# A turn in front of TensorE's attention loop that steps over its body, with six stretches of it under a condition on the counter

## The reference

```python
for t in range(S):
    cur = np.einsum('bhd,bhe->bhde', u[None] * kt, vt)
    y[:, :, t] = np.einsum('bhd,bhde->bhe', rt, state + cur)
    state = w[None, :, :, None] * state + np.einsum('bhd,bhe->bhde', kt, vt)
```

## Time and profile before

| what | value |
|---|---|
| median of 3 runs | 616.07 us (615.64 to 616.73) |
| profiled execution | 615.47 us |
| its span, first to last instruction | 613.7 us |
| mean granted TensorE clock | 0.996 |
| TensorE busy | 596.3 us, 97% |
| VectorE, ScalarE, GpSimd busy | 291.8, 227.6, 145.4 us |
| instruction packets | 29 on q8, 0.48 MB; 12 on q14, 0.10 MB |

### The profile page before, as it was taken

How to read it: one execution, slowest core, us unless ns; L and a number is a source line. 1 busy time by engine, 2 the same in 40 slices (tenths; PEclk the granted TensorE clock), 3 DMA queues, 4 the chain that set the end, 5 groups by cost and what they waited for, 6 DMA issues and landing times.

```text
span 613.7 us, 17314 instructions
## 1 busy us (share of the span) xinstructions
PE 596.3 (97%) x7377; PEld 533.0 (87%) x7377; DVE 291.8 (48%) x462; ACT 227.6 (37%) x409; POOL 145.4 (24%) x177
## 2 busy tenths in 40 slices
PE   6789999999999999999999999999999999999997
PEld 6689999766999999999688888888898888888886
DVE  5578898196677777774121332232132133223212
ACT  3256666434655555552321222132132122213212
POOL 6567887235055332221230000000000000000000
PEclk9899999999999999999999999999999999999999
DMA  7679997595566777640400030030011001001001
GB/s 134 129 150 185 185 184 194 199 321 210 175 240 260 280 273 266 225 148 20 162 1 0 1 104 0 1 103 1 1 51 52 1 1 52 0 1 51 1 0 52
DMA packets 103673, 67.77 MB, mean 110 GB/s; under 512 B 79124, under 2 KB 97688, under 8 KB 103632
## 3 DMA queue, kind: packets, MB, share of 16 engines
q1 hardware_dynamic: 76288, 57.89, 30.9%
q10 hardware_dynamic: 25552, 4.72, 4.1%
q0 software_dynamic: 1792, 4.58, 2.1%
HBM read 55.92 MB, written 12.19 MB: 111 GB/s over the span
## 4 chain that ended last, share of the span: by engine, by line
PE 50%; DVE 0%; ACT 0%; issue 0%
PE gl_pab L1518 32%; PE gl_po L1533 8%; PE p_pair L1533 8%; PE gl_pab L1506 1%; PE p_pair L93 0%; DVE gl_g_lo L1600 0%; DVE gl_g_sb L1598 0%; ACT gl_g_hi L1578 0%; ACT gl_a_sb L1575 0%; DVE gl_o_sb L1611 0%
## 5 line engine op out<-in xcount | busy, mean ns | idle before, releaser
L1598 DVE TENSOR_TENSOR gl_g_sb<-gl_a_sb,gl_pab 128x512 f32<-128x512 f32 x48 | 33.0, 688 | 186.3 <-ACT gl_a_sb L1575 186.3
L1518 PE MATMUL gl_pab<-gl_xT_hi,wm_lo 128*128 128x512 f32 x288 | 112.9, 392 | 0.0
L1518 PE MATMUL gl_pab<-gl_xT_lo,wm_hi 128*128 128x512 f32 x288 | 112.8, 392 | 0.0
L1518 PE MATMUL gl_pab<-gl_xT_hi,wm_hi 128*128 128x512 f32 x288 | 112.1, 389 | 0.0
L1575 ACT ACTIVATE gl_a_sb<-gl_pab 128x512 f32<-128x512 f32 x48 | 28.7, 597 | 183.9 <-PE gl_pab L1518 183.9
L1518 PEld LDWEIGHTS gl_pab<-gl_xT_hi,wm_lo 128*128 128x128 f32 x288 | 54.0, 188 | 11.4
L1518 PEld LDWEIGHTS gl_pab<-gl_xT_hi,wm_hi 128*128 128x128 f32 x288 | 54.1, 188 | 10.6 <-DVE gl_xT_lo L1605 0.3
L1518 PEld LDWEIGHTS gl_pab<-gl_xT_lo,wm_hi 128*128 128x128 f32 x288 | 54.0, 188 | 10.5
L1275 PE MATMUL ex_ph<-ex_xT_hi,ew_w_hi 128*128 128x224 f32 x192 | 52.9, 275 | 0.0
L1275 PE MATMUL ex_ph<-ex_xT_hi,ew_w_lo 128*128 128x224 f32 x192 | 52.7, 274 | 0.0
L1275 PE MATMUL ex_ph<-ex_xT_lo,ew_w_hi 128*128 128x224 f32 x192 | 52.7, 274 | 0.0
(11 more groups left out here) (204 smaller groups left out, 1220.9 us busy)
## 6 DMA issues: line engine op xcount, KB each, us to landing
w_in<-in_moe_w SPq DMA_DIRECT2D x8, 1536.0 KB, 8.1
ew_w_in<-in_moe_w SPq DMA_DIRECT2D x8, 1536.0 KB, 6.5
w_in<-in_moe_w SPq DMA_DIRECT2D x14, 512.0 KB, 7.3
k_in<-in_k SPq DMA_DIRECT2D x48, 96.0 KB
v_in<-in_v ACTq DMA_DIRECT2D x48, 96.0 KB
r_in<-in_r SPq DMA_DIRECT2D x48, 96.0 KB
w_in<-xbuf SPq DMA_DIRECT2D x12, 384.0 KB, 3.8
out<-gl_o_sb SPq DMA_DIRECT2D x12, 384.0 KB, 2.4
```

What stands on the lines that cost most here:

```text
L1518: m = pe.matmul(p_ab[f % 2][w][:, :], a[:, w * KD + k, cols], b[t.slot][:, k, :], start=(k == 0 and n == 0), stop=(k == KD - 1 and n == 2))
L1598: dve.tensor_tensor(g_sb[f % 2][:, :], a_sb[f % 2][:, :], p_ab[f % 2][1][:, :], ALU.mult).then_inc(s_g, 1)
```

## The change

TensorE's loop gets seven turns instead of six. In the turn with c = 0 its body is not run: six stretches of it stand under `pe.If(c > 0)`. Two things that stood ahead of the loop move into that turn, under `pe.If(c < 1)`: the key powers, behind the fourth stretch, and the first tile's transposes with their three waits, at the turn's end. In the other turns the counter is one more than before; so BASE and the initial counts of the semaphores for v grow with it, on all engines, and the waits' constants too. The other engines' loops stay as they are.

```diff
-        BASE = 4
+        BASE = 8
...
-                wait(pe, s_vin[t.slot], t.chunk(32, 64))
+                wait(pe, s_vin[t.slot], t.chunk(32, 96))
...
-            for a in range(2):
-                pe.wait_ge(s_rev, a + 3)
-                for m in range(HP):
-                    i = pe.transpose(p_Y[:, a, m * P:(m + 1) * P], k_rev[a][:, m, :, :].rearrange("p j c -> p (j c)"), ident[:, :])
-                i.then_inc(s_kpT, 1)
-            pe.wait_ge(s_pad, 5)
-            pe.wait_ge(s_zero, ZEROED)
-            pe.wait_ge(s_gates, 32)
+
+            def key_powers():
+                for a in range(2):
+                    pe.wait_ge(s_rev, a + 3)
+                    for m in range(HP):
+                        i = pe.transpose(p_Y[:, a, m * P:(m + 1) * P], k_rev[a][:, m, :, :].rearrange("p j c -> p (j c)"), ident[:, :])
+                    i.then_inc(s_kpT, 1)
+
+            def first_turns():
+                pe.wait_ge(s_pad, 5)
+                pe.wait_ge(s_zero, ZEROED)
+                pe.wait_ge(s_gates, 32)
+                for f, shift in parts[FIRST_TURNS:]:
+                    f(Tile(0, -1, shift))
...
-            schedule(pe, ((natural, -2), (logits, -4), (inputs_ready, -1), (from_states, -1), (own_rows, -1), (updates, -1), (other_rows, -1),
-                          (scores, 0), (turns_ready, 1), (k_transposes, 1), (x_transposes, -2), (r_transposes, 1)), 1, 4, extra, 0, NCH - 1, (turns_ready, x_transposes))
+            parts = ((natural, -2), (logits, -4), (inputs_ready, -1), (from_states, -1), (own_rows, -1), (updates, -1), (other_rows, -1),
+                     (scores, 0), (turns_ready, 1), (k_transposes, 1), (x_transposes, -2), (r_transposes, 1))
+            INPUTS, OTHER, SCORES, FIRST_TURNS = 2, 6, 7, 8
+
+
+            cuts = ((0, 0), (0, OTHER), (1, INPUTS), (1, SCORES), (2, INPUTS), (2, SCORES), (NS, 0))
+            with pe.Fori(0, NCH + 1) as c:
+                for (j, q), end in zip(cuts, cuts[1:]):
+                    with pe.If(c > 0):
+                        while (j, q) != end:
+                            f, shift = parts[q]
+                            f(Tile(c, j - NS, shift))
+                            j, q = (j, q + 1) if q + 1 < len(parts) else (j + 1, 0)
+                    if end == (2, INPUTS):
+                        with pe.If(c < 1):
+                            key_powers()
+                with pe.If(c < 1):
+                    first_turns()
+            schedule(pe, parts, -NT, 4, extra, NCH, NCH - 1, (turns_ready, x_transposes))
...
-                act.sem_inc(x, 32)
+                act.sem_inc(x, 64)
...
-                wait(pool, s_vin[t.slot], t.chunk(32, 64))
+                wait(pool, s_vin[t.slot], t.chunk(32, 96))
```

## The result

The kernel with the change takes 625.88 us (median, 625.22 to 626.21), the kernel before 616.40 beside it: a ratio of 1.0154 [1.0142, 1.0166], slower by 9.5 us. The profiled execution took 625.77 (span 624.0), 10.3 more than the one before.

The account below looks back on a forecast made before the run. The prediction took TensorE to bound the kernel, busy 596.3 of 613.7 us. Its terms, +11.0 - 7.0 - 0.5 + 5.0 = +8.5, gave a median of 624.6 us, range 617 to 631.

Parts of the forecast that it names:

- One to one behind the loop: Behind the attention loop TensorE has no idle time to spare, so any shift of the loop's end passes wholly into the span.
- The walk, +11.0: TensorE's jumps through the added turn fetch code blocks in four rounds; first transposes begin at 20.6 us instead of 9.65.
- up to another 3.9: Extra us at the last jump, if the jumped-over sixth block is fetched ahead of the seventh.
- What a round is: Time from one block fetch to the next on TensorE: mean 4.3 us, only about 1.0 of it the packet.
- Key powers in the walk, 0: Key powers begin at 12.4 instead of 7.14 us, still covered by first transposes at 20.6; cost 0.
- The gaps, -7.0: Five issue gaps in the loop's first turn, 7.04 us, vanish because all blocks are loaded when the first real turn begins.
- the rest, -0.5: Other engines' catching up in the first turn can happen during the walk: -0.5 us (0 to -2.3).
- The conditions, +5.0: Eight conditions in each real turn, six falling through and two jumped over: 0.85 us a turn, six turns (0 to 11).
- 48 branches at 108 ns: Cross-check of the conditions' cost from the Trainium skill's compare-and-branch price of about 108 ns: 5.2 us.
- Residence: The loop's code lies in seven blocks on TensorE, and once loaded all seven stay for the later turns.
- Rival 4: Jumps break the residence of the blocks, so gaps return in every turn: over 650 us; chance 0.02.
- Rival 1, overlapping requests: Jumps ask for targets at once, packets about 1 us apart, first transposes at 10: 614.0, down to 609; chance 0.15.

## Why the prediction held, step by step

- **One to one behind the loop.** Held for this edit: +10.26 at the loop's end, +10.3 in the profiled execution.
- **The walk, +11.0.** It was +12.2. The start was right (the register move was issued at 3.3 where 3.4 was forecast, the second block entered at 3.9 where 3.8 was), and so was the count of four rounds. Their sum was right by luck: 3.85, 4.23 and 3.41 are 1.4 less than three times 4.3, and the last, taken as one of 3.87, was 5.22; together 16.7 where 16.8 was forecast. The last is longer because it passes over the sixth block, which is fetched all the same, beside the seventh. The prediction had that as "up to another 3.9"; it is 1.3. The missing 1.2 lies in what the forecast set at nothing: 0.1 at the start, 0.7 between the rounds (the most of it the short jump of 0.22 inside the fourth block and the issuing of the key powers) and 0.5 from the end of the last branch, at 21.3, to the first transposes.
- **What a round is.** Forecast: 1.0 packet, the rest reaction. Without loads beside it a round is still 3.0, so the loads lengthen a round by 0.4 to 1.1, and moving them doesn't remove the rest.
- **Key powers in the walk, 0.** Held; they began at 12.55 (12.4 forecast) at half clock, and nothing waited for k_dec at 21.84.
- **The gaps, -7.0, and the rest, -0.5.** All gaps went. With its conditions the first turn is 7.27 shorter; without the 1.0 for these it is 8.2 against 7.5 forecast. The 0.7 more isn't the clock, which was low for 3.4 us of this turn before and 3.8 after; what it is stays open. In exchange the 22 transposes ahead of it take 0.49 more at half clock, which no term had.
- **The conditions, +5.0.** 5 turns gave 4.85, so with the first about 5.8: 1.0 a turn where 0.85 was forecast. Three readings held: branches that fall through are 67 to 77 ns, taken ones 209 to 215; the k_dec wait vanished; and the waits stand where the forecast put its two largest items, 0.33 to 0.39 behind the pair of conditions and 0.20 to 0.26 at the turn's head. Six conditions cost 0.65 and the two jumps 0.4. That 48 branches at 108 ns give nearly the same sum is chance: no branch of these turns takes 108, and the four-stretch kernel pays 0.2 a turn for six of them.
- **Residence.** Rival 4 fell: no code packet from 24.5 to 120 us. The prediction weighed the rule of the Trainium skill ("Runtime: NRT & Kernel Launch", "Instruction fetch mechanics") that only two lines exist. It read the section too narrowly: the same section gives TensorE 128 KiB, 2048 instructions, which at its 256 to a block is eight blocks. The traces refute the two lines for TensorE and agree with the eight: the loop's seven stayed in both kernels. No run here has a loop of more. That a taken branch out of what is loaded waits for the fetch is what every jump of the walk to a block not yet there shows, with 3.4 us and more (3.0 without loads). Five packets had begun before the first transposes, where six or seven were forecast.
- **Rival 1, overlapping requests,** has a grain of truth: when a jump passes over one block the two packets run side by side, and the two fetches take 5.2 together and not 7.1. A block is asked for when the one before it is entered: without loads the packet of the fifth begins 0.74 us after the fourth was entered and only 0.17 after the jump to it. So by the time of the last jump the sixth has been asked for, and the jump asks for the seventh besides. Over five blocks it is false: the jump over all was quick only because the blocks weren't fetched.

Terms against measured: +11.0/+12.2, none/+0.5, -7.5/-8.2, +5.0/+5.8; sums +8.5/+10.3. Three small errors of one sign and one of the other; none changes the mechanism.

## What to carry to other kernels

On TensorE, code that is run for the first time comes in blocks, one after another (here 3.0 us for each round, and 3.4 to 4.2 beside loads); fetching ahead of need only gains when the engine has other work in that time, and here TensorE began its work 12 us later to save 8. A condition inside a settled loop is paid every turn, here about 0.1 us each and 0.2 when it jumps, so a one-time gain must be weighed against all turns; the place of the cuts matters more than their number (1.0 a turn became 0.2). Any edit of the code moves the block borders of all that follows, and behind the loop this alone cost 1 to 7 us in these runs: look at the "issue" waits behind the edit before its own time is believed.

## What was not expected of the hardware

- A jump over one block keeps that block for later (5.2 to 5.8 us for both, no gap when it is run); a jump over five fetches none of them, and eight packets are moved instead of six, with gaps of up to 2.79 us behind it.
- The first turn is touchier than its gaps alone. The rows below are TensorE's windows of the first turn in the kernel before, in the run with x first and in the one with six conditions: the idle time fell from 7.1 to 5.4 and 5.0 us, but the busy time rose from 17.23 to 19.19 and 21.40 (0.65 of the last is the conditions). The clock was at 0.50 for 3.4, 10.2 and 13.7 us of it. The run with the loop's head moved lies between, with 18.18 and 6.8. So an estimate from these four is 0.3 us of first turn for each us at the lower level. No run changed the clock alone.

```profile
10.36:34.69 24.33, 17.23 (x735) 15.75 (x732) 11.41 (x20) 5.13 (x10) 14.73 (x16) 0.93 0.77 145
...
10.03:34.58 24.55, 19.19 (x732) 17.84 (x730) 11.44 (x20) 5.13 (x10) 14.98 (x16) 0.79 0.79 153
...
9.91:36.32 26.41, 21.40 (x731) 19.82 (x730) 11.81 (x21) 5.10 (x10) 15.32 (x16) 0.74 0.72 138
```

- No variant was faster than the kernel before. Three ended the loop 0.3 to 0.5 us earlier in their one profiled execution, no more than executions of one kernel differ by (615.4 to 618.0 for the kernel before), and each met one new wait for code behind the loop (1.3, 1.8 and 4.1 us).
